# One round trip of the softmax reciprocals per head pair, P.V one step later, one weight-sum store one pair earlier, in a fused attention and two-FFN kernel

## The reference

```python
scores = q @ k.T / 8, causal                       # per head, 576 x 576
a = exp(scores - max);  a /= a.sum(-1) + 1e-9
local = a @ v
q_p = phi(q)                                       # elu + 1
mem_out = (q_p @ M_prev) / (q_p . z_prev + 1e-6)
g = sigmoid(beta)
x = g * mem_out + (1 - g) * local                  # 2304 x 512
x = (silu(x @ w_gate) * (x @ w_val)) @ w_out       # first network
h = x @ w_in
y = where(h >= 1, h, where(h <= -1, 0, (h + 1)**2 / 4)) @ w_out2
```

## Time and profile before

| what | value |
|---|---|
| median of 3 runs | 1056.67 us (1054.94 to 1058.01) |
| the profiled execution | 1057.46 us |
| its span, first to last instruction | 1055.6 us |
| mean granted TensorE clock | 0.984 |
| busy share of the span: PE, DVE, ACT, POOL | 94%, 75%, 54%, 48% |
| attention, from the start to the last `out_x` | 0 to 229.1 us |
| networks | 229.1 to 1055.6 us |

### The profile page before, as it was taken

How to read it: one execution, slowest core, us unless ns; L and a number is a source line. 1 busy time by engine, 2 the same in 40 slices (tenths; PEclk the granted TensorE clock), 3 DMA queues, 4 the chain that set the end, 5 groups by cost and what they waited for, 6 DMA issues and landing times.

```text
span 1055.6 us, 19322 instructions
## 1 busy us (share of the span) xinstructions
PE 996.4 (94%) x6344; PEld 924.9 (88%) x6344; DVE 788.1 (75%) x1454; ACT 569.2 (54%) x1146; POOL 505.7 (48%) x407
## 2 busy tenths in 40 slices
PE   5999968988999899999899999999999999999998
PEld 3776645677999899999799999999899999899997
DVE  5776758925767766677676778878898789988776
ACT  4877866845544544545445445545465455654551
POOL 4554656607667622346322357565662344632321
PEclk8999998999999999999999999999999999999999
DMA  5343432314333233332323323323413423135111
GB/s 204 129 146 128 135 131 94 121 63 140 126 114 100 101 100 109 131 101 81 99 101 132 127 80 100 121 65 116 131 70 120 136 104 120 60 121 172 69 41 61
DMA packets 44129, 116.17 MB, mean 110 GB/s; under 512 B 7665, under 2 KB 16001, under 8 KB 44033
## 3 DMA queue, kind: packets, MB, share of 16 engines
q1 hardware_dynamic: 44032, 114.93, 32.2%
HBM read 100.16 MB, written 14.75 MB: 109 GB/s over the span
## 4 chain that ended last, share of the span: by engine, by line
PE 77%; DVE 7%; issue 6%; DMA 3%; ACT 3%; POOL 2%; SPq 1%; DVEq 0%; ACTq 0%; POOLq 0%
PE ps L1278 23%; PE ps L1280 22%; PE ps L1279 22%; PE ps L1233 4%; PE ps L1202 3%; PE ps L1261 3%; DMA rsums<-rrow 2%; DVE xt_l L970 1%; DMA nat<-nat_in 1%; DVE xy L1084 1%; DVE hid_r L1074 1%; DVE tmp L1068 1%; ACT wu_h L703 1%; DVE negs L897 1%; ACT rown L671 1%
## 5 line engine op out<-in xcount | busy, mean ns | idle before, releaser
L581 POOL TENSOR_TENSOR wu_l<-wu_r,wu_h 128x768 fp32r<-128x768 f32 (+1 forms) x75 | 140.9, 1886 | 410.8 <-ACT wu_h L703 410.8
L1278 PE MATMUL ps<-xt_h,wu_h 128*128 128x384 f32 x840 | 284.1, 338 | 19.2 <-DVE xt_l L970 10.1
L1280 PE MATMUL ps<-xt_h,wu_l 128*128 128x384 f32 x840 | 282.1, 336 | 0.0
L1279 PE MATMUL ps<-xt_l,wu_h 128*128 128x384 f32 x840 | 282.1, 336 | 0.0
L1278 PE MATMUL ps<-hid_h,wd_h 128*128 128x384 f32 x672 | 227.5, 338 | 7.7 <-DVE xy L1084 7.5
L1279 PE MATMUL ps<-hid_l,wd_h 128*128 128x384 f32 x672 | 225.8, 336 | 0.0
L1280 PE MATMUL ps<-hid_h,wd_l 128*128 128x384 f32 x672 | 225.8, 336 | 0.0
L1084 DVE TENSOR_TENSOR xy<-xy,ps 128x384 f32<-128x384 f32 x288 | 157.9, 549 | 58.7 <-PE ps L1280 57.8
L771 ACT ACTIVATE hid_h<-hid_r 128x768 fp32r<-128x768 f32 x84 | 70.9, 844 | 211.9 <-DVE hid_r L1058 156.5
L1278 PEld LDWEIGHTS ps<-xt_h,wu_h 128*128 128x128 f32 x840 | 158.5, 189 | 25.8 <-issue 25.6
L1279 PEld LDWEIGHTS ps<-xt_l,wu_h 128*128 128x128 f32 x840 | 158.6, 189 | 0.0
(11 more groups left out here) (85 smaller groups left out, 1343.0 us busy)
## 6 DMA issues: line engine op xcount, KB each, us to landing
wu_r<-w_up SPq DMA_DIRECT2D x60, 512.0 KB, 4.7
wd_r<-w_down SPq DMA_DIRECT2D x42, 512.0 KB, 3.8
wu_r<-kept SPq DMA_DIRECT2D x38, 512.0 KB, 5.6
qk<-qk_in SPq DMA_DIRECT2D x16, 640.0 KB, 4.5
kept<-wu_r SPq DMA_DIRECT2D x19, 512.0 KB, 4.2
nat<-nat_in SPq DMA_DIRECT2D x16, 384.0 KB, 5.0
vm<-vm_in SPq DMA_DIRECT2D x16, 320.0 KB, 3.3
rbc<-rsums SPq DMA_DIRECT2D x64, 64.0 KB, 2.6
```

The lines of the kernel that those rows point to most:

```text
L581: nc.gpsimd.tensor_tensor(wu_l[u % 3][:, a:b], wu_r[u % 3][:, a:b], wu_h[u % 2][:, a - 1:b - 1].bitcast(F32), ALU.subtract).then_inc(low_p ...
L1278: nc.tensor.matmul(dst, w_hi, v_hi, start=start, stop=False, skip_group_check=onto)
L1279: nc.tensor.matmul(dst, w_hi, v_lo, start=False, stop=False, skip_group_check=onto)
L1280: return nc.tensor.matmul(dst, w_lo, v_hi, start=False, stop=stop, skip_group_check=onto)
```

## The change

VALUES becomes 6, EVAC_A 8, EVAC_B 7, KEEP 10. There is one `sums_inverse` per pair over all nine columns (VectorE, one step after tile 1), one transpose, one copy, and rsums has one contiguous row of 576 numbers per head. Two writes bring it there: 8 rows of 512 bytes, and one row of 2 x 256 bytes for the first block. Two reads of 64 partitions x 2304 bytes bring it back. SP loads q, k and row-wise q before v. `v_scale` moves from steps with j % 4 = 2 to j % 4 = 3.

```diff
-    EXP, MEMS, TURN, VALUES, EVAC_A, EVAC_B = 1, 1, 3, 5, 7, 6
+    EXP, MEMS, TURN, VALUES, EVAC_A, EVAC_B = 1, 1, 3, 6, 8, 7
-    KEEP = 11
+    KEEP = 10
-        rrow, a = place("rrow", [P, 2, 2, P], F32, a)
+        rrow, a = place("rrow", [P, 2, P], F32, a)
-        rsums = nc.dram_tensor("rsums", [NPAIR, NBLK, P], F32, kind="Internal").ap()
+        rsums = nc.dram_tensor("rsums", [NPAIR, 2, S], F32, kind="Internal").ap()
...
+        def ends_pair(j, g):
+            return tile_of(j)[1] == 1 and g == 1
+        def r_rows(j):
+            return ps[0:NBLK, group_bank(j, 1), 2 * P:3 * P]
...
+            def write_r(p):
+                sp.wait_ge(r_row, p + 1)
+                sp.dma_start(rsums[p, :, D:].rearrange("h (i n) -> i h n", n=P), rrow[1:NBLK, p % 2]).then_inc(r_out, 16)
+                sp.dma_start(rsums[p:p + 1, :, 0:D], rrow[0:1, p % 2].rearrange("o (h n) -> o h n", h=2)).then_inc(r_out, 16)
+            def read_r(p):
+                sp.wait_ge(r_out, 32 * (p + 1))
+                at_least(sp, x_done, 2 * (p - 1))
                 for h in range(2):
+                    sp.dma_start(rbc[D * h:D * h + D, p % 2], rsums[p, h:h + 1].broadcast_to([D, S])).then_inc(r_in[p % 2], 16)
...
             for p in range(1, NPAIR):
-                if p > 1:
-                    load_v(p)
                 if 1 < p and p + 1 < NPAIR:
                     load_qk(p + 1)
                 if p + 2 < NPAIR:
                     load_nat(p + 2)
-                for part in range(2):
-                    write_r(p - 1, part)
-                    read_r(p - 1, part)
+                if p > 1:
+                    load_v(p)
+                write_r(p - 1)
+                read_r(p - 1)
                 if p == KEEP:
                     keep_sums(1)
...
-                if k == 2 and p < NPAIR:
+                if k == 3 and p < NPAIR:
...
+            def sums_inverse(p):
+                at_least(dve, expd, 2 * SLOTS * (p + 1))
+                at_least(dve, expdf, p + 1)
+                nc.vector.tensor_scalar(den[:, p % 2], rsum[:, p % 2], 1e-9, None, ALU.add).then_inc(dend, 1)
+                at_least(dve, dend, p + 1)
+                at_least(dve, turned, groups_before(SLOTS * (p - 1)))
+                nc.vector.reciprocal(rden[:, p % 2], den[:, p % 2]).then_inc(rdend, 1)
...
-                at_least(dve, r_in[part][p % 2], (32, 64)[part] * (p // 2 + 1))
+                at_least(dve, r_in[p % 2], 32 * (p // 2 + 1))
...
-                if MEMS <= j < NSTEP + MEMS:
-                    sums_inverse(j - MEMS)
+                if MEMS <= j < NSTEP + MEMS and tile_of(j - MEMS)[1] == 1:
+                    sums_inverse(tile_of(j - MEMS)[0])
...
+                    if ends_pair(j, g):
+                        pe.wait_ge(rdend, p + 1)
+                        mm = nc.tensor.transpose(r_rows(j), rden[:, p % 2], ident[:])
```

More of the change, by code:

```diff
@@ L145, in attention_two_ffns @@
         ld_v = [sem(f"ld_v{s}") for s in range(2)]
-        r_in = [[sem(f"r_in{part}{s}") for s in range(2)] for part in range(2)]
+        r_in = [sem(f"r_in{s}") for s in range(2)]
         r_row = sem("r_row")
@@ L373, in attention_two_ffns @@
         SCORE_F = 1024
-        R_BLOCKS = (slice(2 * SLOTS - 3, NBLK), slice(0, 2 * SLOTS - 3))
-        def r_part(i, g):
-            return {(2, 1): 0, (1, 1): 1}.get((i, g))
-        def r_rows(j, g):
-            part = r_part(tile_of(j)[1], g)
-            k = R_BLOCKS[part]
-            a, b = GROUPS[tile_of(j)[1]][g]
-            col = (b - a) * P
-            return slice(0, k.stop - k.start), slice(col, col + P)
+        def ends_pair(j, g):
+            return tile_of(j)[1] == 1 and g == 1
+        def r_rows(j):
+            return ps[0:NBLK, group_bank(j, 1), 2 * P:3 * P]
         def out_place(i):
@@ L487, in _ @@
                     load_nat(p + 2)
-                for part in range(2):
-                    write_r(p - 1, part)
-                    read_r(p - 1, part)
+                if p > 1:
+                    load_v(p)
+                write_r(p - 1)
+                read_r(p - 1)
                 if p == KEEP:
                     keep_sums(1)
-            for part in range(2):
-                write_r(NPAIR - 1, part)
-                read_r(NPAIR - 1, part)
+            write_r(NPAIR - 1)
+            read_r(NPAIR - 1)
             for u in range(STEPS):
@@ L686, in copy_pt @@
                     at_least(act, turned, groups_before(j) + g + 1)
-                    part = r_part(tile_of(j)[1], g)
-                    if part is not None:
+                    if ends_pair(j, g):
                         p = tile_of(j)[0]
-                        rows, cols = r_rows(j, g)
-                        at_least(act, r_out, 16 * (2 * p + part - 3))
-                        nc.scalar.activation(rrow[rows, part, p % 2], ps[rows, group_bank(j, g), cols], ACT.Copy).then_inc(r_row, 1)
+                        at_least(act, r_out, 32 * (p - 1))
+                        nc.scalar.activation(rrow[0:NBLK, p % 2], r_rows(j), ACT.Copy).then_inc(r_row, 1)
                     dst, src = group_ends(j, g)
@@ L917, in mem_scale @@
                                                ALU.add, ALU.mult).then_inc(mscaled, 1)
-            def sums_inverse(j):
-                p, i = tile_of(j)
-                if i not in (3, 1):
-                    return
-                part = 0 if i == 3 else 1
-                k = R_BLOCKS[part]
-                at_least(dve, expd, 2 * (j + 1))
-                if i == 1:
-                    at_least(dve, expdf, p + 1)
-                nc.vector.tensor_scalar(den[:, p % 2, k], rsum[:, p % 2, k], 1e-9, None, ALU.add).then_inc(dend, 1)
-                at_least(dve, dend, 2 * p + part + 1)
+            def sums_inverse(p):
[3 more added lines that the diff above has]
+                at_least(dve, dend, p + 1)
                 at_least(dve, turned, groups_before(SLOTS * (p - 1)))
-                nc.vector.reciprocal(rden[:, p % 2, k], den[:, p % 2, k]).then_inc(rdend, 1)
+                nc.vector.reciprocal(rden[:, p % 2], den[:, p % 2]).then_inc(rdend, 1)
             def copy_pt(j):
@@ L1234, in turn @@
                                                  rown[:, j % ROWN, col:col + P], ident[:])
-                    part = r_part(i, g)
-                    if part is not None:
-                        rows, cols = r_rows(j, g)
-                        pe.wait_ge(rdend, 2 * p + part + 1)
-                        mm = nc.tensor.transpose(ps[rows, group_bank(j, g), cols], rden[:, p % 2, R_BLOCKS[part]], ident[:])
+                    if ends_pair(j, g):
+                        pe.wait_ge(rdend, p + 1)
+                        mm = nc.tensor.transpose(r_rows(j), rden[:, p % 2], ident[:])
                     mm.then_inc(turned, 1)
```

15 lines of the change are left out of this document (removed).

## The result

The changed kernel takes 1037.5 us in the median, against 1056.05 us for the kernel before on the same chip: a ratio of 0.9828 with a 95% interval of 0.9809 to 0.9847. Five of its six runs lie between 1036.98 and 1038.66 us; one, at a granted clock of 0.56, took 1618.59 and is not compared. The profiled execution is the one of 1036.98 us, with a span of 1034.9 us. The forecast was 1038, the range 1034 to 1046, so the number is right. The sum behind it is right in its large terms, off in several small ones, and about 1 us came in a stretch for which it has no term.

A forecast was written before the change was run, and what follows sets the result against it. TensorE bounds ordinary pairs; SP's ring, the late store's stall and VectorE bound three stretches. Terms 1.0 + 0.2 + 0.8 + 2.5 + 0.8 + 10.7 + 1.6 + 1.4 = 19.0 off 1057.46 gave 1038.5, stated as 1038; range 1034 to 1046.

The forecast's parts named there:

- one transpose of 0.11 us goes: Every pair: one of two transposes of reciprocals goes; 1.0 us over TensorE-bound pairs 2 to 10, 0.2 in the last two.
- P.V's fill: Start of attention: with P.V a step later, TensorE reaches the steady pairs without one P.V block, gaining 0.8 us.
- SP's ring: Pairs 7 to 10: SP's closed loop of two round trips, about 12 us, sets the pace; removing one gains 2.5 us.
- The cover of 2.8 us: Each pair: reads land at 14.1 us, VectorE asks at 16.9, so the single round trip costs nothing.
- The slower rival: The single round trip exceeds its cover and stalls 15 pairs; a write landing at 7.5 us gives 1061; chance 0.03.
- The store: Pair 11: issuing the weight-sum store a pair earlier removes VectorE's 12.25 us stall, less 1.5 for GpSimd contention; net 10.7.
- VectorE's removed work: VectorE-bound stretch of three pairs: one add and one reciprocal less per pair, worth 1.0 us, taken as 0.8.
- Pair 14: From the scores of pair 14 to those of pair 15: a gain of 0.1 us.
- The end: Last reciprocals to last out_x: earlier transpose, fewer reads and a faster write landing gain 1.6 us (1.2 to 2.0).
- No gap before the fourth product: Networks' start: TensorE's 2.77 us gap closes and its clock stays up, gaining 1.4 us (0 to 1.65).
- The change touches nothing after the last `out_x`: Only the first 229 us of the span can move, apart from how TensorE starts into the networks.

The follow-up runs named there:

- the changed kernel's second run: The changed kernel run again, unaltered, beside the kernel with earlier weight sums on another chip; 1037.14 us, 0.9823 to the kernel before.
- Experiment 3: The kernel before with only P.V and both out_x one step later (VALUES 6, EVAC_A 8, EVAC_B 7); 1058.54 us, 1.0021.
- Experiment 7: The kernel before with P.V and out_x a step later and KEEP 10, keeping two round trips and the old load order; 1045.64 us, 0.9902.
- experiment 4: The changed kernel with P.V and out_x set back a step (VALUES 5, EVAC_A 7, EVAC_B 6); 1039.14 us, 0.984.
- experiment 5: The changed kernel with the load of v back ahead of the loads of q, k and row-wise q; 1037.16 us, 0.9828.
- experiment 6: The changed kernel with a pair's two reads cut into six, same bytes, the last pair keeping two; 1036.95 us, 0.9822.
- The runs with the early sums: The changed kernel with GpSimd's three sets of weight sums in steps 26, 30 and 34, run twice; 1035.24 us (0.9808) and 1035.35 us (0.9805).
- experiment 10: The changed kernel with weight sums in steps 26, 30, 34 and GpSimd's input sums and high parts also spread over steps; 1034.96 us, 0.9805.
- experiment 1: The kernel before with only the store of the weight sums one pair earlier (KEEP 10 for 11); 1044.83 us, 0.9889.

## Why the prediction was right, and where it was not

- **TensorE bounds the ordinary pair; one transpose of 0.11 us goes.** Right: 11.47 us a pair.
- **P.V's fill, 0.8.** Right, as far as the scatter lets one say. The stretch to pair 2 gained 1.8: 0.8 from pair 1 to pair 2 (12.45 to 11.61), where the block is missing, and 1.0 before the scores of pair 1 (21.62 to 20.65). The second part is scatter of the start: in the traces of this study these scores start between 20.7 and 21.9 us, the changed kernel's second run at 21.7. Over all thirteen traces the scores of pair 2 start at 33.0 us in the mean with P.V six steps behind (32.3 to 33.7) and at 34.0 with five (33.8 to 34.2). Experiment 3 adds a condition: alone, the step later isn't a gain at all, since the wait for the store takes it back.
- **SP's ring, 2.5 (0 to 2.9).** All 2.9: the stretch gained 3.9, less 1.0 for the transposes. Experiment 7, which puts two trips back but keeps P.V's step, loses 1.9 there beside the transposes, and not by the reads: a load of q and k comes late.
- **The cover of 2.8 us.** Right to 0.2 at either end, and experiments 4, 5 and 6 take from it, each in another way. P.V's step takes all of it and makes three waits of 1.1 us together; the later landing of the write leaves 1.2 us, the longer issue of the reads 0.9, and neither makes a wait in the ordinary pairs. The slower rival needed a write landing in 7 us; the changed kernel's SP waited 0.9 us for it at most.
- **The store, 12.25, less 1.5 for GpSimd.** Mechanism and place are right (135.94 and 142.80 for 136.5 and 143). Where I said 10.7 and 0.8 for VectorE's removed work, 10.7 came in all, and pair 14 gave back 0.4. With the 0.8 at its full size the contention was 2.3 (12.25 + 0.8 - 10.7), or 2.7 with pair 14: above my 1.5. By its size it is near the 2.9 to which the rule of the Trainium skill ("SBUF — State Buffer", the contention on the engine side) would come here; but the trace shows other instructions of GpSimd than the four sums among those that block, so the two numbers don't measure the same. The runs with the early sums get 1.3 of it back in this stretch, 1.8 by the medians. The granted clock in the last 21.6 us of the stretch averages 0.92 in both traces of the changed kernel, and 1.00 in both with the early sums, which none of my terms held. VectorE's idle time in the stretch is the same with either (2.4 and 2.3 us), so the traces show no loss by the clock beside it.
- **Pair 14, 0.1.** It lost 0.4. All four traces with two round trips have 11.6 us there. Those with one have 11.9 to 12.0, except experiment 10, which spreads the preparation of the inputs and has 11.5. So the two meet there; which instruction makes the loss is open.
- **The end, 1.6 (1.2 to 2.0).** This term was mis-sized: 0.75 came, with 1.7 predicted together with the transpose. The 0.8 up to the last write are right (0.85). The saving behind it, 0.4 for one transfer less in line and 0.4 for a landing with nothing in flight, didn't come (-0.1). Two writes cost 0.67 and 0.61 us of issue where I had taken 0.5 for each, from a row of a simpler pattern, and the reads, now 144 KB each, needed 3.1 us from the last issue to the landing (208.28 to 211.39 in the chain of waits) where I had 2.6 from 64 KB. How large the shortfall is remains unsure: other traces have 25.8 us in this stretch with two trips (experiments 1 and 7) and 24.3 with one (the changed kernel's second run), which would be 1.5.
- **No gap before the fourth product.** Wrong: 1.47 us remained. But it was enough: the clock stayed, for 1.5 us where I had 1.4.
- **"The change touches nothing after the last `out_x`".** Not quite: the first 35 us of the networks are 1.0 us shorter with one round trip, beside the clock, and the cause is open.

So the total met the number partly because small errors cancel: +1.0 at the start, +0.4 in the ring, +0.1 in the clock and +1.0 in the networks against 0.8 in pairs 11 to 13, 0.5 in pair 14 and 0.9 at the end leave +0.3; and the sum was made against an execution that lay above the median. That part is luck. The mechanism of the large terms, the store and SP's ring, is not.

How the 18.6 us divide can only be said with the order in which the parts are taken. The store alone brings 11.6, and 6 to 7 as the last part. The round trip with its order of loads brings 8.5 as the last part, some 2.5 of it because the store is late without it. P.V's step loses 2 us alone and seems to gain some 1.6 as the last part, with intervals that overlap. The store and the round trip both shorten the same wait, and P.V's step pays only once this wait no longer sets the time.

## What to carry to other kernels

Where one queue issues write, wait, read, wait in a closed ring, add up issues and serial landings and compare the sum with the time of a round: what lies below it is free (six reads in place of two changed nothing once one landing was gone), what lies above it is paid in every round and in everything that the queue issues later. One round trip less, with its transpose, changed 8.5 us here, and only part of that in waits for the data of the trip itself. A stall whose end is set by another queue's program is cut by shortening or reordering that program; a head start of the waiting engine doesn't help until then. Where a wait is for several semaphores, look at when each of them came: the view named GpSimd for a wait that was the store's. And a stall is often where another engine works undisturbed: when it goes, look at what that engine now holds up, and move it to where the bound is elsewhere.

## What the runs showed of the hardware

**The clock after a short gap.** TensorE's idle time ahead of the fourth product, with the granted clock of the next 2 to 4 us:

| gap, us | clock after it | kernel |
|---|---|---|
| 1.27 | 1.00 | the change without the store |
| 1.47 | 1.00 | the changed kernel |
| 2.54 | 0.70 | the change with P.V as it was |
| 2.62 | 0.50 | P.V later alone |
| 2.73 | 1.00 | the change without the single round trip |
| 2.77 | 0.50 | before |
| 3.30 | 0.55 | the store alone |

The 0.50 is the 1.2 GHz level; a mean between the two is a window that holds both. The gaps of up to 1.5 us cost nothing in any trace. Of five gaps of 2.5 to 3.3 us four brought the clock down and one didn't. Shorter ones can do it too: a gap of 2.4 us in pair 12 was followed by a clock of 0.50 in both traces of the changed kernel (2.43 us up to 159.90, 0.50 by 160.2) and in experiment 5, but not in experiment 1; and one of 2.0 us, at 345 us in the changed kernel, in eight of the thirteen traces. Of the five at the start of the networks, the rows of the one that didn't and of the first experiment, the store alone:

```profile
220.20:223.50 3.30, 3.27 (x19) 3.30 (x20) 1.02 (x2) 0.97 (x3) 0.00 (x0) 1.00 0.81 211
```

```profile
219.20:222.00 2.80, 2.80 (x10) 2.80 (x11) 0.44 (x1) 0.73 (x2) 0.00 (x0) 0.55 0.77 214
```

Nineteen products in 3.3 us against ten in 2.8. A term for the clock behind such a gap is therefore a chance and not a sum, and with 1.4 to 1.6 us, by the same products in the four traces that lost it, it is as large as many edits.

**Small writes.** The second write has two pieces of 256 bytes. At the end, with little else in flight, the writes had landed 1.59 us after the issue of the second began, of which 0.61 was the issue; in the pairs SP waited 0.9 us at most after issuing it. The rule of the Trainium skill ("DMA: Bandwidth & Descriptors", specifications) that pieces under 512 bytes make the DMA engine read, modify and write, which I had weighed, shows no cost here that these rows could tell.

**Issue times differ by pattern.** In the pair shown above SP's issue took 0.33 us for v, 0.53 for q and k, 0.42 for the next load, 1.13 for two broadcast reads, and 0.68 and 0.63 for the two writes, where the write of before took 0.49. For a queue that sets the end these are terms to look up one by one.
